# TensorE's instruction stream written out for all rounds: a loop of 15 iterations replaced by straight-line code

## What is computed

```
w = weight_gen - np.max(weight_gen, axis=-1, keepdims=True)
w = np.exp(w)
w = w / (np.sum(w, axis=-1, keepdims=True) + 1e-09)
out = np.einsum('bshk,bskhg->bshg', w, x_unf)      # 7 taps, x padded in front by 6 tokens

h = x @ w_in                                       # 16384 x 192 times 192 x 2048
relu6 = np.clip(h + 3.0, 0.0, 6.0)
g = h * relu6 / 6.0
return (g @ w_out)                                 # 16384 x 2048 times 2048 x 192
```

## Time and profile before

| | us |
|---|---|
| median of 3 runs | 1243.03 |
| lowest, highest | 1239.11, 1248.18 |
| the profiled execution | 1239.38 |
| its span, first to last instruction | 1236.6 |
| mean granted TensorE clock in it | 0.985 of full speed |
| TensorE busy in it | 1170.4 |

### The profile page before, as it was taken

One profiled execution on the slowest core, in us unless ns is written; L12 is line 12 of the kernel. 1 busy time (PEld: TensorE's weight loads), 2 busy tenths in 40 slices (PEclk: granted clock), 3 DMA queues, 4 the chain that ended last, 5 costly groups with the idle time before them and its releaser, 6 DMA issues.

```text
span 1236.6 us, 33823 instructions
## 1 busy us (share of the span) xinstructions
PE 1170.4 (95%) x13696; PEld 1095.7 (89%) x13696; DVE 818.9 (66%) x1362; ACT 662.4 (54%) x1269; POOL 691.1 (56%) x455
## 2 busy tenths in 40 slices
PE   1999999999999999999999999999999999999998
PEld 1898998989989898998989989899898989989997
DVE  7866766657666666666667666676666666666664
ACT  3554555545555455455555555555454555555553
POOL 7793671927639085490936719276390854909300
PEclk9999999999999999999999999999999999999999
DMA  6101010010100101001010100101001010010000
GB/s 177 46 22 59 20 48 15 22 60 21 47 15 22 60 22 59 2 29 52 22 60 16 52 15 22 60 22 58 3 22 60 22 59 2 27 54 14 15 15 14
DMA packets 12203, 44.25 MB, mean 36 GB/s; under 512 B 1183, under 2 KB 5279, under 8 KB 10139
## 3 DMA queue, kind: packets, MB, share of 16 engines
q1 hardware_dynamic: 12059, 41.93, 9.7%
HBM read 29.34 MB, written 12.58 MB: 34 GB/s over the span
## 4 chain that ended last, share of the span: by engine, by line
PE 92%; DVE 3%; ACT 2%; issue 1%; POOL 1%; DMA 0%; DVEq 0%; ACTq 0%
PE sums L548 32%; PE work L512 16%; PE work L526 13%; PE sums L551 13%; PE work L527 9%; PE work L513 7%; DVE g_lo L362 2%; DVE work L357 1%; ACT g_hi L266 1%; ACT relu L261 1%; PE work L477 1%; PE work L464 1%; POOL pool_acc L166 0%; POOL pool_prod L164 0%; DVE w_in L413 0%
## 5 line engine op out<-in xcount | busy, mean ns | idle before, releaser
L548 PE MATMUL sums<-w_out,g_hi 64*128 64x384 f32 x4096 | 649.7, 357 | 2.8 <-DVE g_lo L362 2.1
L551 PE MATMUL sums<-w_out,g_lo 64*128 64x192 f32 x4096 | 558.4, 249 | 0.0
L357 DVE SCALAR_TENSOR_TENSOR work<-relu,work 128x512 f32<-128x512 f32 x512 | 331.2, 693 | 331.1 <-ACT relu L261 329.8
L261 ACT ACTIVATE relu<-work 128x512 f32<-128x512 f32 x512 | 279.4, 601 | 400.6 <-PE work L527 398.2
L548 PEld LDWEIGHTS sums<-w_out,g_hi 64*128 64x128 f32 x4096 | 438.4, 186 | 19.8 <-issue 3.1
L551 PEld LDWEIGHTS sums<-w_out,g_lo 64*128 64x128 f32 x4096 | 442.9, 189 | 0.2
L266 ACT CAST g_hi<-work 128x512 fp32r<-128x512 f32 x512 | 300.9, 588 | 76.0 <-DVE work L357 73.6
L362 DVE TENSOR_TENSOR g_lo<-work,g_hi 128x512 fp32r<-128x512 f32 x512 | 330.1, 687 | 14.4
L159 POOL TENSOR_TENSOR pool_acc<-x_in,w_soft 128x768 f32<-128x768 f32 (+1 forms) x32 | 50.0, 1562 | 461.4 <-DVE w_soft L351 454.6
L166 POOL TENSOR_TENSOR pool_acc<-pool_acc,pool_prod 128x768 f32<-128x768 f32 (+1 forms) x160 | 295.6, 1847 | 0.0
L512 PE MATMUL work<-xt_a,w_in 64*128 64x512 f32 x768 | 235.7, 414 | 35.9 <-DVE g_lo L362 28.1
(11 more groups left out here) (47 smaller groups left out, 960.4 us busy)
## 6 DMA issues: line engine op xcount, KB each, us to landing
x_in<-x_dram SPq DMA_DIRECT2D x15, 1344.0 KB, 6.0
out_dram<-out_stage SPq DMA_DIRECT2D x32, 384.0 KB, 3.0
w_raw<-weight_gen_dram SPq DMA_DIRECT2D x16, 224.0 KB, 3.0
w_out_raw<-moe_w_out_dram SPq DMA_DIRECT2D x1, 1152.0 KB, 13.3
x_in<-x_dram SPq DMA_DIRECT2D x1, 768.0 KB, 5.0
w_in_raw<-moe_w_in_dram SPq DMA_DIRECT2D x1, 768.0 KB, 8.1
w_in_raw<-moe_w_in_dram SPq DMA_DIRECT2D x2, 384.0 KB, 10.1
w_out_raw<-moe_w_out_dram SPq DMA_DIRECT2D x1, 384.0 KB, 6.2
```

The costliest lines, as they stand in the source:

```text
L261: nc.scalar.activation(t.relu[:, m % 2, :], t.work[m % BANKS][:], ACT.Relu, bias=3.0).then_inc(s.relu_ready, 1)
L357: nc.vector.scalar_tensor_tensor(bank[:], t.relu[:, m % 2, :], 6.0, bank[:], ALU.min, ALU.mult).then_inc(s.gated, 1)
L548: nc.tensor.matmul(t.sums[n][:, 0:2 * D], t.g_hi[rows, m % G_SLOTS, n * P:(n + 1) * P], t.w_out[rows, j, :], start=(j == 0 and part == 0), ...
L551: ins = nc.tensor.matmul(t.sums[n][:, D:2 * D], t.g_lo[rows, m % G_SLOTS, n * P:(n + 1) * P], t.w_out[rows, j, 0:D], start=False, stop=las ...
```

## The change

One line. TensorE's loop over q is run when the program is built, so its body stands in the stream 15 times, one behind the other, with q a constant in each.

```
@@ tensor_program
     pe.wait_ge(s.w_out_lo, 2)
 
-    with pe.Fori(0, PAIRS - 1) as q:
+    for q in range(PAIRS - 1):
         for d in range(FIRST_DUO + 1, FIRST_DUO + 1 + DUOS):
             duo(q, d)
```

## The result

| | before | change |
|---|---|---|
| median us (runs) | 1244.03 (4) | 1187.20 (4) |
| lowest to highest | 1239.11 to 1248.18 | 1186.77 to 1189.02 |
| ratio to before, 95% interval | | 0.9547 (0.951 to 0.9585) |
| profiled execution, its span | 1239.38, 1236.6 | 1189.02, 1187.2 |

What follows compares the result with a forecast made beforehand. The prediction took PE (TensorE), busy 1170.4 us, to set the pace, with stops at its loop ends. 1239.4 less 33.3 (stops), 2.2 (lost overlap) and 13.5 (clock) gave 1190.4, so 1191 us expected, range 1185 to 1206.

Steps and rivals of the forecast that it cites:

- The branch: At TensorE's loop end, taken 14 times: idle stretches of 33.3 us and 2.2 us of lost overlap go, together 35.5 us.
- comparison with 108 ns a branch: At the loop end, rival: 14 branches of about 108 ns worth 1.5 us, giving 1237.9 us; chance of no change 0.05.
- The clock: PE's clock halved behind nine of the 14 loop-end stops, 1.50 us each; these go with the stops, 13.5 us.
- The registers: Register instructions in TensorE's loop, 61 and 22 an iteration, hide behind the matmuls: 0, upper bound 6 us.
- Fetch: Instruction fetch of TensorE's straight-line code stays hidden, cost 0; rival that it stalls PE: slower, up to 1442 us, chance 0.03.
- What is late next: VectorE's idle time behind its softmax step shrinks from 5.68 to about 1.3 us, the thinnest cover; it still waits for TensorE.
- The sum: Whole kernel: 1239.4 - 33.3 - 2.2 - 13.5 = 1190.4 us, against the profiled execution.
- no clock row under 1.00 after the first 40 us: Sign of being right, in the trace's clock rows: PE's granted clock stays full after the first 40 us.
- The spread: Over the kernel's runs: 3.6 us between profiled execution and median come from halvings and stop lengths; less spread after.

Runs made afterwards that it cites:

- e4: The change plus, at each of the 14 former loop ends, a two-iteration loop with one semaphore increment as body; 1190.97 us, ratio 0.9583.
- e1: The kernel before, TensorE's loop kept but its branch announced with `hint_back_edge=True`; 1189.29 us, ratio 0.9581.
- e5: The change, with TensorE waiting at the 14 former loop ends for duo 20's last `g_lo`, needed a duo later; 1227.40 us, ratio 0.9903.
- e2: The kernel before with TensorE's loop written out but q kept in a register, 1230 register instructions remaining, no branch; 1189.48 us, ratio 0.9577.
- r1: The change unaltered, timed again on one chip beside the hinted loop and the kernel before; 1189.83 us, ratio 0.9577.
- e7: The change, with the loops of the other four engines (ScalarE, VectorE, GpSimd, SyncE) written out as well; 1190.47 us, ratio 0.9595.

## Why the prediction was right

It said 1191 us, from 1185 to 1206, with 0.92 on faster by over 1%; measured were 1187.2 and, again, 1189.8.

**The branch.** 35.5 us for 14 stops and their lost overlap. The trace after has none of the stops, and the difference in idle time alone is 33.5 us. The place was right, and so was the reading against the profile's own label, which had named `g_lo` 12 times of 14. What decided it was to ask which tile L512 really waits for, and to find it ready before PE ran dry. The record of the branch itself, 3.3 to 4.0 us long at each of the 14 places, was in the trace of the kernel before and settles it; the prediction did not use it and came to the cause by exclusion. The prediction blamed "the branch"; e4 and e1 make that more exact: it is the far target, unannounced. Its comparison with 108 ns a branch is loose: the idle stretches are 18 to 25 times that and not everywhere "more than 20 times", and the branch itself lasts over 30 times that.

**The clock.** 13.5 us for nine halvings. Busy time in the 15 rounds fell by 16.6 us, of which 2.2 us is the lost overlap; that leaves 14.4 us for the clock, 0.9 us more than forecast, which the wandering of the rounds covers. That it goes with idle time and not with the jump was an argument then and is shown by e5.

**The registers.** Taken as 0, bound 6 us; e2 shows 0.75 us in 15 rounds, not told from 0.

**Fetch.** Taken as hidden; the change fetches 92 packets in 980 us where the loop fetched 117, and no stop follows. Forecast were about 110 in all, it is 107. The prediction took the size that the Trainium skill gives for TensorE's instruction memory, 2048 instructions (Runtime: NRT & Kernel Launch, section Instruction fetch mechanics), concluded that the loop would run without fetches, and set this aside since the loop fetches all the time. That conclusion is the prediction's own and not the section's. For the plain loop the trace was right, but e1 shows that a body of 1,797 instructions does stay when the branch is announced. The size agrees with e1; the plain loop doesn't profit from it.

**What is late next.** VectorE's cover was to shrink to about 1.3 us; it is 1.17 us in the first round.

**The sum.** 1190.4 us against the profiled execution, 1189.0 measured. It missed by 1.4 us, and rounds of 71.5 in place of 71.8 us make up to 4.5 us in 15, so nothing finer can be read from the sum. The one thing that went a little the other way is the prologue: PE's stop there, 2.11 us in the earlier trace rows, was 3.19 us in the change, and the clock halved behind it until 41.6 us, so the sign "no clock row under 1.00 after the first 40 us" was missed by that much.

**The spread.** The prediction put the 3.6 us between profiled execution and median down to the number of halvings and the length of the stops. The 11 runs of before beside r1 bear this out in size: the fastest, 1236.30 us, had a granted clock of 0.989, the slowest, 1245.21 us, one of 0.981, and 0.008 of 1240 us is 9.9 us against 8.9 measured. With the stops gone the spread halves. The profiled execution of before was the fastest of its four, so the medians gained more, 56.8 us, than the 52 us that the prediction's 1191 stood for.

## What to carry to other kernels

Where an engine that is otherwise always busy stops once per iteration, find which value the first instruction of the loop needs; if it was ready in time, suspect the loop's jump, and count the stop and what the clock loses behind it. Writing the loop out and announcing the branch were worth the same here, and the second keeps the program short and, where the body fits, saves the fetches. Look at the branch's own record in the trace before anything else. Here the branches and registers of engines with slack were worth nothing (e7), and so were the registers in TensorE's stream (e2), which is worked ahead of the array.

## What the runs showed of the hardware that had not been expected

- A loop body of 1,797 instructions on TensorE runs for 980 us without one instruction packet when its closing branch is announced; without the hint the loop moves 117 packets in the same 980 us, 9 in each iteration for a body of 7.
- A taken branch of TensorE's sequencer lasts 3.3 to 4.0 us with a far target, 0.22 to 0.26 us with the same target announced, and 0.21 to 0.23 us with a near one; work already issued covers the first 1.4 to 1.5 us.
- With a body of three rounds the announced jump still leaves 0.35 to 0.75 us of stop, against 2.16 to 2.40 us unannounced.
- TensorE's clock fell to half behind 5 of 14 stops of 1.7 us and behind none of 14 of 1.1 us, with the same work between them, each in one execution. Stops of 2.5 to 3.0 us in four prologues had no halving behind them.
- A round of the same 856 matmuls, PE busy and at full clock, takes 71.4 to 72.1 us; an execution may hold only rounds of 71.5 us, or nearly only such of 71.8.
